# Attention probabilities split in place and turned by a transposing DMA, in a fused attention and two-layer MoE kernel on one core

## What is computed

```
attention: 4 batches, 8 heads, 576 positions, head size 64, scores / 8,
           block-causal mask of 64 x 64 blocks (query block i sees key blocks 0..i),
           softmax over keys, times v                        -> x, 2304 x 512
layer 1:   h = x @ w_in (512 x 1024); solu = h * softmax(h);
           layer norm * g_ln; @ w_out (1024 x 512)           -> 2304 x 512
layer 2:   h = x @ w_in (512 x 2048); g = h * tanh(softplus(h)) ("mish");
           g @ w_out (2048 x 512)                            -> 2304 x 512
```

## Time and profile before

| | |
|---|---|
| median of 3 runs | 745.59 us (742.27 to 747.0) |
| the profiled execution | 743.46 us |
| its span, first to last instruction | 741.6 us |
| PE busy | 714.2 us (96%) |
| DVE busy | 469.2 us (63%) |
| ACT busy | 397.3 us (54%) |
| POOL busy | 167.6 us (23%) |
| DMA queue q1 | 50.1% of 16 engines, 109.08 MB |
| mean granted TensorE clock | 0.995 |

### The profile page before, as it was taken

One profiled execution on the slowest core, in us unless ns is written; L12 is line 12 of the kernel. 1 busy time (PEld: TensorE's weight loads), 2 busy tenths in 40 slices (PEclk: granted clock), 3 DMA queues, 4 the chain that ended last, 5 costly groups with the idle time before them and its releaser, 6 DMA issues.

```text
span 741.6 us, 17885 instructions
## 1 busy us (share of the span) xinstructions
PE 714.2 (96%) x7300; PEld 549.7 (74%) x7300; DVE 469.2 (63%) x992; ACT 397.3 (54%) x832; POOL 167.6 (23%) x273
## 2 busy tenths in 40 slices
PE   9989999999899999999999999999999999987996
PEld 8567865777467867886788688866787678856885
DVE  5997678455844786558746886577357843770271
ACT  5787865466735563456635663566256633551240
POOL 5450301452544101720311023402120110000000
PEclk9999999999999999999999999999999999999999
DMA  8265336565575429641935076516513482228537
GB/s 315 88 170 186 138 100 144 165 181 198 143 190 191 141 69 253 185 121 46 240 109 159 25 220 191 163 36 179 142 38 122 139 224 67 64 84 207 172 107 234
DMA packets 114208, 110.21 MB, mean 149 GB/s; under 512 B 43472, under 2 KB 95696, under 8 KB 114128
## 3 DMA queue, kind: packets, MB, share of 16 engines
q1 hardware_dynamic: 114128, 109.08, 50.1%
HBM read 86.51 MB, written 13.11 MB: 134 GB/s over the span
## 4 chain that ended last, share of the span: by engine, by line
PE 78%; DVE 8%; DMA 7%; ACT 3%; issue 1%; POOL 1%; SPq 1%; ACTq 0%; DVEq 0%; POOLq 0%
PE banks L1047 23%; PE banks L1099 12%; PE banks L1029 12%; PE banks L1016 9%; PE banks L964 5%; PE banks L989 5%; PE banks L1069 4%; PE banks L950 4%; PE banks L1110 3%; DMA lnT<-ln_split 2%; DMA t_raw<-w 2%; DVE solu L1224 2%; DMA own<-w 2%; DVE stat L1215 1%; DMA wo<-wd 1%
## 5 line engine op out<-in xcount | busy, mean ns | idle before, releaser
L855 POOL TENSOR_SCALAR prob<-prob,rinv 128x64 f32<-128x64 f32 (+8 forms) x144 | 86.0, 609 | 362.8 <-DVE rinv L1177 362.7
L1047 PE MATMUL banks<-x2T_hi,WH 128*128 128x256 f16 x576 | 157.1, 273 | 0.0
L1047 PE MATMUL banks<-x2T_lo,WH 128*128 128x256 f16 x576 | 157.0, 273 | 0.0
L1047 PE MATMUL banks<-x2T_hi,WL 128*128 128x256 f16 x576 | 157.0, 273 | 0.0
L1099 PE MATMUL banks<-wo,gT_hi 128*128 128x256 f16 x784 | 143.7, 273 | 10.2 <-DVE stat L1226 5.2
L1397 ACT ACTIVATE pT_hi<-banks 128x512 f16<-128x512 f32 (+2 forms) x128 | 64.0, 501 | 123.5 <-PE banks L964 98.1
L1183 DVE TENSOR_TENSOR pT_lo<-banks,pT_hi 128x512 f16<-128x512 f32 (+2 forms) x128 | 73.1, 571 | 83.8 <-ACT pT_hi L1397 83.0
L1099 PE MATMUL banks<-wo,gT_lo 128*128 128x256 f16 x392 | 106.8, 273 | 0.0
L1029 PE MATMUL banks<-lnT,WH 128*128 128x256 f16 x576 | 98.7, 276 | 4.9 <-DMA lnT<-ln_split 4.9
L1387 ACT ACTIVATE prob<-banks,nmax 128x64 f32<-128x64 f32 (+8 forms) x144 | 74.7, 523 | 49.9 <-DVE nmax L1171 39.1
L1099 PEld LDWEIGHTS banks<-wo,gT_hi 128*128 128x128 f16 x784 | 76.6, 98 | 25.4 <-DVE stat L1226 6.6
(11 more groups left out here) (115 smaller groups left out, 1302.4 us busy)
## 6 DMA issues: line engine op xcount, KB each, us to landing
wo<-wd SPq DMA_DIRECT2D x196, 256.0 KB, 4.0
w_raw<-w SPq DMA_DIRECT2D x11, 512.0 KB, 6.0
out<-own SPq DMA_DIRECT2D x36, 128.0 KB, 3.1
q_raw<-q SPq DMA_DIRECT2D x16, 256.0 KB, 4.1
wd<-wo_first SPq DMA_DIRECT2D x16, 256.0 KB, 4.5
t_raw<-w SPq DMA_DIRECT2D x8, 512.0 KB, 4.1
wd<-t_split SPq DMA_DIRECT2D x8, 512.0 KB, 4.9
wo_second<-wd SPq DMA_DIRECT2D x8, 512.0 KB, 4.9
```

What stands on the lines that cost most here:

```text
L855: pool.tensor_scalar(of, of, rinv[:, u % 2, i:i + 1], S_X, ALU.mult, ALU.mult).then_inc(norm_done, 1)
L1047: mm = pe.matmul(banks[:, MI_BANK[n % 2], G * j:G * (j + 1)], w2i(b, c, m), (x2T_hi, x2T_lo)[a][:, c], start=(c == 0 and i == 0), stop=(c ...
```

## The change

- POOL no longer normalises. `invert` makes the reciprocal and, in a second DVE instruction, 64 / sum (`rinv`).
- `high` (ACT) now reads `prob` in SBUF, scales by `rinv` and writes the high half, block by block (144 instructions in place of 128); `low` (DVE) does prob * rinv - high, block by block (144 in place of 128). Both halves lie in `halves`, untransposed, high half first, in two rooms.
- `turn` goes from PE to SP: one DMA transpose per unit (80), of 2 x `all_columns(u)` float16 columns: 4, 8, 12, 16 and 10 blocks of 128x128 for tiles 0 to 4, 800 blocks in all. It waits for `low` and the zeroed columns of its unit and for `values` of unit u - 2. `values` waits for its landing.
- `prob` has one room instead of two; `exps` of a unit waits for `low` of the unit before. `zero_columns` writes both halves and waits for the landing of unit u - 2. The bank that held transposes is now a second bank for `values`.
- `v_raw` has one room instead of two: each load of v waits for the split of the load before.
- All times in `TIMES` are new. In the new order the first `solu_out` comes after `values` of units 0 to 12, `score` of units 0 to 15 and two parts of `solu_in` of the next group (before: `values` 0 to 11, `score` 0 to 13, none). There are 156 `warm` transposes again, in 10 places, all of them before `score` of unit 8. Between `score` of unit 25 and its `values` PE has `score` 26 and 27, `values` 24 and one part of `solu_in` (6 matmuls of 512 columns); between `score` 26 and `values` 26 it has `score` 27, `values` 24 and 25 and four parts of `solu_in`. Apart from these, unit 27 and the units of the start up to 12, only units 63 and 67 have under 8 us of PE work between `score` and `values`.

```diff
--- before
+++ after
-S_BANK, T_BANK, O_BANK = 0, 2, 3
+S_BANK, O_BANK = 0, 2
...
+def padded(u):
+
+    return P * chunks_of(place(u)[1])
+
+
+def all_columns(u):
+    return padded(u) * len(blocks_of(place(u)[1]))
...
-    return BC if a == 1 else O_BANK
...
+    return O_BANK + a % 2
...
-WARM = (33, 17, 6, 15, 6, 3, 3, 9, 21, 23, 18, 2)
-WARM_EARLY = 8
+WARM = (33, 17, 8, 23, 4, 30, 9, 8, 3, 21)
+WARM_EARLY = 10
...
-        v_raw = sb("v_raw", [P, 2, KCH, P], F32)
+        v_raw = sb("v_raw", [P, KCH, P], F32)
...
-        prob = sb("prob", [P, 2, 1024], F32)
-        pT_hi, pT_lo = sb("pT_hi", [P, 2, 8, P], F16), sb("pT_lo", [P, 2, 8, P], F16)
+
+        prob = sb("prob", [P, 1024], F32)
+        halves = sb("halves", [P, 2, 2048], F16)
+        pT = sb("pT", [P, 2, 16, P], F16)
...
             def load_v(n):
-                wait(sp, v_lo_done, keys_split(n - 2) if n >= 2 else 0)
+                wait(sp, v_lo_done, keys_split(n - 1) if n >= 1 else 0)
                 c = FIRST_KEYS // P if n < PAIRS else 0
-                sp.dma_start(v_raw[:, n % 2, c:4].rearrange("r c n -> r (c n)"), va[n, :, P * c:512]).then_inc(v_in[n % 2], 16)
-                sp.dma_start(v_raw[0:64, n % 2, 4], vb[n]).then_inc(v_in[n % 2], 16)
+                sp.dma_start(v_raw[:, c:4].rearrange("r c n -> r (c n)"), va[n, :, P * c:512]).then_inc(v_in, 16)
+                sp.dma_start(v_raw[0:64, 4], vb[n]).then_inc(v_in, 16)
...
+            def turn(u):
+                z, n = u % 2, 2 * all_columns(u)
+                sp.wait_ge(p_lo_done, subs(u + 1))
+                sp.wait_ge(pad_done, pads(u))
+                wait(sp, pv_done, u - 1)
+                sp.dma_start(pT[:, z, 0:n // P], halves[:, z, 0:n], transpose=True).then_inc(turned[z], 16)
...
             def zero_columns(u):
                 b, tile, p = place(u)
-                wait(pool, pT_done, turns(u - 1) if u else 0)
-                at = width(blocks_of(tile)[0])
-                pool.memset(prob[:, u % 2, at:at + BLOCK], 0.0).then_inc(pad_done, 1)
-
-            def normalise(u):
-                b, tile, p = place(u)
-                pool.wait_ge(rinv_done, u + 1)
-                for i, blk in enumerate(blocks_of(tile)):
-                    of = prob[:, u % 2, 512 * i:512 * i + width(blk)]
-                    pool.tensor_scalar(of, of, rinv[:, u % 2, i:i + 1], S_X, ALU.mult,
-                                       ALU.mult).then_inc(norm_done, 1)
+                wait(pool, turned[u % 2], 16 * (u // 2))
+                at, n = width(blocks_of(tile)[0]), all_columns(u)
+                both = halves[:, u % 2, 0:2 * n].rearrange("r (a n) -> r a n", a=2)
+                pool.memset(both[:, :, at:at + BLOCK], 0.0).then_inc(pad_done, 1)
 
...
-            def turn(u, rnd):
-                b, tile, p = place(u)
-                n = turns(u) + rnd
-                if rnd == 0:
-                    pe.wait_ge(norm_done, subs(u + 1))
-                    pe.wait_ge(pad_done, pads(u))
-                wait(pe, pT_lo_done, t_before(n) + 1)
-                for at, (i, c) in enumerate(blocks_turned(tile)[4 * rnd:4 * rnd + 4]):
-                    mm = pe.transpose(banks[:, t_bank(n), P * at:P * (at + 1)],
-                                      prob[:, u % 2, 512 * i + P * c:512 * i + P * (c + 1)], ident[:])
-                mm.then_inc(pT_done, 1)
             def values(u):
...
-                    wait(pe, x_lo_done, o_before(a) + 1)
-                pe.wait_ge(pT_lo_done, turns(u + 1))
-                for c in range(chunks_of(tile)):
-                    for term, (vv, pp) in enumerate(((v_hi, pT_hi), (v_lo, pT_hi), (v_hi, pT_lo))):
+                    wait(pe, x_lo_done, a - 1)
+                pe.wait_ge(turned[z], 16 * (u // 2 + 1))
+                n, of_heads = chunks_of(tile), pT[:, z].rearrange("r s (h n) -> r (s h) n", h=2)
+                for c in range(n):
+                    for term, (vv, part) in enumerate(((v_hi, 0), (v_lo, 0), (v_hi, 1))):
                         for h in range(2):
                             cols = slice(DH * h, DH * (h + 1))
-                            halves = pp[:, z].rearrange("r s (h n) -> r (s h) n", h=2)
+                            at = 2 * (part * n * len(blocks_of(tile)) + c) + h
                             if tile == 4:
-                                of = pp[:, z, c, cols]
-                            elif in_quarters(u):
-                                of = halves[:, 4 * c + h:4 * c + 4 - h:3 - 2 * h]
+                                of = of_heads[:, at]
                             else:
-                                of = halves[:, 4 * c + h:4 * c + 4:2]
+                                step = 2 * n + (1 - 2 * h if in_quarters(u) else 0)
+                                of = of_heads[:, at:at + step + 1:step]
                             mm = pe.matmul(banks[DH * h:DH * (h + 1), o_bank(a), nq * p:nq * (p + 1)], vv[:, p, c, cols], of,
                                            start=(c == 0 and term == 0),
                                            stop=(c == chunks_of(tile) - 1 and term == 2), skip_group_check=True)
...
             def invert(u):
-                n = len(blocks_of(place(u)[1]))
+                z, n = u % 2, len(blocks_of(place(u)[1]))
                 dve.wait_ge(exp_done, subs(u + 1))
-                dve.reciprocal(rinv[:, u % 2, 0:n], rsum[:, u % 2, 0:n]).then_inc(rinv_done, 1)
-
-            def low(u, rnd):
-                n = turns(u) + rnd
-                size = len(blocks_turned(place(u)[1])[4 * rnd:4 * rnd + 4])
-                dve.wait_ge(pT_hi_done, n + 1)
-                dve.tensor_tensor(pT_lo[:, u % 2, 4 * rnd:4 * rnd + size].rearrange("r a n -> r (a n)"),
-                                  banks[:, t_bank(n), 0:P * size],
-                                  pT_hi[:, u % 2, 4 * rnd:4 * rnd + size].rearrange("r a n -> r (a n)"),
-                                  ALU.subtract).then_inc(pT_lo_done, 1)
+                dve.reciprocal(recip[:, z, 0:n], rsum[:, z, 0:n]).then_inc(recip_done, 1)
+                dve.wait_ge(recip_done, u + 1)
+                dve.tensor_scalar(rinv[:, z, 0:n], recip[:, z, 0:n], S_X, None, ALU.mult).then_inc(rinv_done, 1)
+
+            def low(u, i):
+                z, at, n = u % 2, padded(u) * i, width(blocks_of(place(u)[1])[i])
+                dve.wait_ge(p_hi_done, subs(u) + i + 1)
+                dve.scalar_tensor_tensor(out=halves[:, z, all_columns(u) + at:all_columns(u) + at + n],
+                                         in0=prob[:, s_place(u, i):s_place(u, i) + n], scalar=rinv[:, z, i:i + 1],
+                                         in1=halves[:, z, at:at + n], op0=ALU.mult, op1=ALU.subtract).then_inc(p_lo_done, 1)
...
                 act.wait_ge(max_done, subs(u) + (2 if u < EARLY else i + 1))
-                if i == 0 and u >= 2:
-                    act.wait_ge(pT_done, turns(u - 1))
+                if u < EARLY:
+                    wait(act, p_lo_done, subs(u - 1) if u >= 2 and i == 0 else 0)
+                elif in_quarters(u) and in_quarters(u - 1):
+                    act.wait_ge(p_lo_done, subs(u - 1) + i + 1)
+                elif i == 0:
+                    act.wait_ge(p_lo_done, subs(u))
                 at = s_place(u, i)
-                act.activation(prob[:, u % 2, 512 * i:512 * i + width(blk)], scores[:, at:at + width(blk)], ACT.Exp,
-                               bias=nmax[:, u % 2, i:i + 1], scale=1.0,
-                               accum_out=rsum[:, u % 2, i:i + 1]).then_inc(exp_done, 1)
-
-            def high(u, rnd):
-                n = turns(u) + rnd
-                size = len(blocks_turned(place(u)[1])[4 * rnd:4 * rnd + 4])
-                act.wait_ge(pT_done, n + 1)
-                if rnd == 0:
-                    wait(act, pv_done, u - 1)
-                act.activation(pT_hi[:, u % 2, 4 * rnd:4 * rnd + size].rearrange("r a n -> r (a n)"),
-                               banks[:, t_bank(n), 0:P * size], ACT.Copy).then_inc(pT_hi_done, 1)
+                act.activation(prob[:, at:at + width(blk)], scores[:, at:at + width(blk)], ACT.Exp, bias=nmax[:, u % 2, i:i + 1],
+                               scale=1.0, accum_out=rsum[:, u % 2, i:i + 1]).then_inc(exp_done, 1)
+
+            def high(u, i):
+                z, at, n = u % 2, padded(u) * i, width(blocks_of(place(u)[1])[i])
+                act.wait_ge(rinv_done, u + 1)
+                if i == 0:
+                    wait(act, turned[z], 16 * (u // 2))
+                act.activation(halves[:, z, at:at + n], prob[:, s_place(u, i):s_place(u, i) + n], ACT.Copy,
+                               scale=rinv[:, z, i:i + 1]).then_inc(p_hi_done, 1)

```

213 lines of the change are left out of this document (97 added, 116 removed), and 242 rows, old and new, of the table TIMES.

## The result

The changed kernel takes **772.56 us** (median of 4 runs, 770.26 to 773.54) against 744.72 us of the kernel before in the same comparison (4 runs, 742.27 to 747.00). The ratio is 1.037, 95% interval 1.033 to 1.041: slower by 28 us. The comparisons further down found 744.7 to 746.3 us for the kernel before, so a difference of 2 or 3 us between kernels of different comparisons is not told from noise. I had predicted 735 us, range 723 to 752, so the sign was wrong and the time outside the range.

What follows compares the result with a forecast made beforehand. The prediction took PE (busy 714.2 of 741.6 us) as the bound. Transposes -42, start +14, waits of `values` +8, SP and DMA +9 gave -11 us: 735 us for the median, range 723 to 752.

Steps and rivals of the forecast that it cites:

- The transposes, -42: After the first `solu_out`, 349 transposes leave PE at 0.12 us each: 42 us saved.
- PE busy near 650 us: A sign that would show the forecast right: PE's total busy time after the change.
- Edits at nothing: `high` on ACT, extra DVE work and single rooms of `prob` and `v_raw` hide behind PE work after the start: 0.
- hidden while units are over 4 us apart: With one room of `prob`, `exps` waits for the `low` before it; claimed to cost nothing at that spacing.
- The start, +14: Before the first `solu_out`: +10 for longer unit chains with DMA landings, +2.4 for DVE, +2 for the clock.
- Waits of `values`, +8: After the start, PE idles for landings: about 5 us at unit 25, 2 at 26 and 27, 1 at 63 and 67.
- SP and DMA, +9: New transposes meet weight loads and stores on SP's queue and the DMA engines, in seven groups: 9 us lost.
- Clock, +2: In the start, longer PE waits bring one more fall to half clock: 2 us, from 0 to 4.
- the third: SP becomes the bound of the last seven groups, `turn` standing between loads of `wo`: 766 us; chance 0.14.
- The fourth: Transposing by DMA is itself too slow, so the queue is the bound: 750 us upward; chance 0.01.
- All ends together +28 or so: Whole run: the forecast's terms all at their unfavourable ends, against -46 with all at the favourable ends.
- wrong if: After the start: the forecast fails if PE is idle for less than 30 us or more than 60.

Runs made afterwards that it cites:

- b_free: Kernel before in its own order, PE transposes of the probabilities left out from unit 8 on, for nothing in their place: 722.09 us, ratio 0.968.
- a_free: Changed kernel without its 80 DMA transposes; `values` reads a piece of `v_hi` and waits for `low` only: 749.86 us, ratio 1.005 to the kernel before.
- f_prob3: Changed kernel's code, nothing turned, three rooms of `prob`, old steps exactly in the order of before: 742.94 us, ratio 0.997 to the kernel before.
- f_prob2: Changed kernel's code, nothing turned, two rooms of `prob`, old steps exactly in the order of before: 756.11 us, ratio 1.014 to the kernel before.
- a_nowait: Changed kernel with all DMA transposes issued, but `values` does not wait for them: 770.37 us, ratio 1.032 to the kernel before.

## Why the prediction was wrong

Measured, the 28 us are a sum of three: the transposes left PE, -23 (b_free); what the new code and order cost with nothing turned, +28 (a_free against b_free); the DMA transposes, +23 (after against a_free). My sum had -42, +4 (VectorE +2.4, clock +2) and +27 (10 in the start, 8 of `values`, 9 of the queue). The parts are taken in two orders, so they need not add up in any other.

By place the same runs tell more. The first `solu_out` and the end of the span are taken from one execution each (before, b_free, a_free, after):

| us | predicted | measured |
|---|---|---|
| start: transposes | 0 | -0.7 (57.4 to 56.7) |
| start: code and order | +4 | +15.2 (to 71.9) |
| start: landings | +10 | +1.8 (to 73.7) |
| behind: transposes | -42 | -19.4 (684.2 to 664.8) |
| behind: code and order | 0 | +10.4 (to 675.2) |
| behind: landings, queue | +17 | +21.2 (to 696.4) |

The new order has some 5 us of PE work ahead of the first `solu_out` that the old one has behind it. They make "start: code and order" dearer by up to that much, and the same row behind the start cheaper.

- **The transposes, -42: the step that failed first.** The count was right and 0.12 us near: PE's busy time fell by 36.6 us for 376 transposes in b_free, 0.10 each. What failed is that "every us of PE work removed there counts, if something is ready to fill the place": 16.5 us came back as idle. I priced the condition at nothing. With -23 my sum would have been +8. It is the largest miss of the six rows, 23 of the 39 us by which they differ in sum. The sign "PE busy near 650 us" took off all 66 us of busy time, against my own reading of 42; 688.7 was measured.
- **"Edits at nothing": the step that failed next.** I hid the one room of `prob`, the second operation and the scaled evictions behind PE work. Behind the start they and the order cost 10.4 us; in the start 15.2, where I had charged 4. The arithmetic (5 us in all) and the room by itself (3 to 6) do not make up the sum; what the rest is, in the new order, no run shows. The sentence "hidden while units are over 4 us apart" looked at the distance between units on PE. The rows show what stands between them on ScalarE and VectorE: exponential, inverse, `high`, `low` and the next exponential alternate between two queues that run in order, and whatever else stands in either (mish, g_low, layer norm) stands in the middle. Before, the unit left that file early: GpSimd normalised it and PE read it, and its room was free. That this is the rest of the cost is argued; f_prob3 shows 13 us of it in the old order.
- **The start, +14.** 16.3 us measured (57.4 to 73.7): right in size by luck, wrong in its parts. With nothing turned it is still at 71.9, so some 2 us hang on landings in that order, not 10; in the old order it is at 65.8 (f_prob2) against 56.7. VectorE, which I charged 2.4 us, is busy 10.5 us longer up to the first `solu_out` (58.0 against 47.5): `low` takes 4.7 more and the second operation 4.3, in part for the two more units that stand there. Here is `low` before, then after, then the second operation:

```profile
L1183 DVE TENSOR_TENSOR pT_lo<-banks,pT_hi 128x256 f16<-128x256 f32 (+1 forms) x16 | 8.8, 552 | 1.9 <-ACT pT_hi L1397 1.7
...
L1146 DVE SCALAR_TENSOR_TENSOR halves<-prob,rinv,halves 128x64 f16<-128x64 f32 (+7 forms) x28 | 13.5, 511 | 4.3 <-ACT halves L1361 4.2
...
L1141 DVE TENSOR_SCALAR rinv<-recip 128x2 f32<-128x2 f32 x15 | 4.3, 289 | 0.5
```

- **Waits of `values`, +8.** PE waits 11.5 us there, 8.0 of them behind the start: the size was right by luck. The longest wait (2.5 us, at 55 us) lies in the start, and at unit 25, where I had put 5 us, there is none; PE waits 4.6 us for exponentials at `score` 26 and 27 instead. And a_nowait shows that these waits are worth next to nothing: take them away and `score` waits. That a late landing is paid through the rooms of `halves` is a path that I had not followed.
- **SP and DMA, +9.** With the two above, the DMAs were put at 27 and measured 23. The size was right for the wrong reason. The landings were read well: the shortest for 4, 8, 12 and 16 blocks were 2.4, 3.0, 3.7 and 4.3 us, as 1.8 us and 0.156 a block give. The DMA engines' share was 70.5%, not 67.
- **Clock, +2.** Nine stretches at half clock instead of the one more that I took, about 17 us of PE time by the estimate above. How much of that is loss in the run is open: filling the three of the start gained 4.5 us, and none of it where they were.

Of the rivals the third came nearest in time, 766 us, and the wrong place: PE waited 5.4 us for wo, where I had asked for 20. The fourth, 750 us upward, holds the time too, but not for its reason: with no block turned by DMA the kernel still takes 749.9 us. "All ends together +28 or so" add up to +31 with 38 us for the transposes; my range stopped at 752 all the same. The "wrong if" of 60 us idle was met: 63.9 us behind 75 us.

The Trainium skill ("VectorE: DVE Perf Modes", Rules for kernel authors) prefers TensorE for a 128x128 transpose whose result may go to PSUM. Its sign was right here. Its price of 1309 ns for one by DMA (The three transpose paths) does not carry over to many: the 80 turns, 64 of them with 8 blocks or more, land in 4.2 us in the median, and those of 16 blocks in 4.3 at least, far from 1.3 us a block.

## What to carry to other kernels

- Work taken from the bounding engine is worth its time only as far as nothing was hiding under it. Before counting it, leave the work out for nothing, as b_free does: it gives the ceiling in one run, and here it was half of the estimate.
- A buffer is held from its writer to its last reader. When a change puts the last reader further down (a copy instead of a direct read, a transfer instead of a matmul), follow who waits for the room, on every in-order engine on the way; here the new wait itself, taken away, gave 2 us of 23.
- An order written for one set of waits is worth little for another: this code, turning nothing and with two rooms of `prob`, takes 756 us in exactly the old order and 747 in its own. A few steps misplaced while carrying an order over cost more than that (17 us), so compare orders only when each is followed exactly.
